# First MLP of an attention and two-MLP kernel: its first products split into 64-row pairs, in two phases with the transposes of an older tile between them

## The reference

```python
# attention: 4 x 8 heads, 576 positions, 64 wide; a score below (max - tau) is dropped
scores = scale * q @ k.T
attn = softmax(where(scores >= max - tau, scores, -1e9))
x = (attn @ v) as 2304 x 512
# first MLP
h = x @ w_in                            # 2304 x 1024
sm = exp(h - max(h)) / (sum + 1e-9)
solu = h * sm
ln = (solu - mean) / sqrt(var + 1e-6) * g_ln
y = ln @ w_out                          # 2304 x 512
# second MLP
h = y @ w_in2                           # 2304 x 2048
out = (max(h, 0) + log1p(exp(-abs(h)))) @ w_out2
```

## Time and profile before

| | |
|---|---|
| Median of 3 runs | 888.11 us (887.92 to 888.94) |
| The profiled execution, its own time | 887.9 us |
| Its span in the trace | 886.2 us |
| Granted TensorE clock, mean over the span | 0.998 |
| Busy: PE, PEld | 861.7 us (97%), 716.5 us (81%) |
| Busy: DVE, ACT, POOL | 638.6 us (72%), 567.1 us (64%), 324.3 us (37%) |
| Products h_ps of line 1040 | 432, in three groups of 144 |
| Transposes of line 1188 | 288 |
| The part with tiles 2 to 17 and their y_ps | about 275.7 to 463.0 us of the span |

### The profile page before, as it was taken

One profiled execution on the slowest core, in us unless ns is written; L12 is line 12 of the kernel. 1 busy time (PEld: TensorE's weight loads), 2 busy tenths in 40 slices (PEclk: granted clock), 3 DMA queues, 4 the chain that ended last, 5 costly groups with the idle time before them and its releaser, 6 DMA issues.

```text
span 886.2 us, 16881 instructions
## 1 busy us (share of the span) xinstructions
PE 861.7 (97%) x6248; PEld 716.5 (81%) x6248; DVE 638.6 (72%) x1286; ACT 567.1 (64%) x1040; POOL 324.3 (37%) x425
## 2 busy tenths in 40 slices
PE   6899999999999999999999999999999999999998
PEld 4566666666667889898899999999999999999996
DVE  6899999999955633615447578867858858868865
ACT  3787988787876533424356566666666667667664
POOL 3554677555544601102021232333332232233232
PEclk9999999999999999999999999999999999999999
DMA  6713423343001100000021500000100000000000
GB/s 167 205 47 81 110 55 75 88 108 108 18 1 37 37 1 1 2 1 1 1 84 49 178 1 1 37 0 1 37 1 1 37 1 1 36 0 0 36 0 36
DMA packets 30394, 37.16 MB, mean 42 GB/s; under 512 B 4720, under 2 KB 18544, under 8 KB 30320
## 3 DMA queue, kind: packets, MB, share of 16 engines
q1 hardware_dynamic: 29920, 35.90, 14.7%
q10 hardware_dynamic: 400, 0.30, 0.1%
HBM read 31.46 MB, written 4.72 MB: 41 GB/s over the span
## 4 chain that ended last, share of the span: by engine, by line
PE 55%; issue 25%; POOL 9%; DVE 9%; ACT 0%; DMA 0%; ACTq 0%; POOLq 0%; DVEq 0%
PE h_ps L1040 12%; PE y_ps L1176 11%; POOL w_lo L527 9%; PE m_ps L1152 8%; PE f_ps L1241 7%; DVE ntop L837 7%; PE s_ps L1072 7%; PE o_ps L1112 5%; PE t_ps L1088 2%; PE lt_ps L1188 1%; PE s_ps L1067 1%; DVE kept L853 1%; DVE inv L869 0%; PE l_ps L1083 0%; DMA k_sb<-k_t 0%
## 5 line engine op out<-in xcount | busy, mean ns | idle before, releaser
L1152 PE MATMUL m_ps<-y_hi,w 128*128 128x384 f32 x768 | 211.8, 337 | 0.0
L527 POOL TENSOR_TENSOR w_lo<-w_rest,w_hi 128x512 fp32r<-128x512 f32 x84 | 110.3, 1313 | 253.5 <-ACT w_hi L700 253.4
L1152 PEld LDWEIGHTS m_ps<-y_hi,w 128*128 128x128 f32 x768 | 140.3, 188 | 3.9
L580 ACT ACTIVATE expd<-s_ps,ntop 128x576 f32<-128x576 f32 x144 | 106.2, 741 | 51.6 <-DVE ntop L837 51.6
L1152 PE MATMUL m_ps<-y_lo,w 128*128 128x384 f32 x384 | 129.0, 336 | 0.0
L700 ACT CAST w_hi<-w_rest 128x512 fp32r<-128x512 f32 x84 | 52.2, 622 | 109.1 <-PE f_ps L1241 105.7
L465 POOL TENSOR_SCALAR kept<-kept,inv 128x576 f32<-128x576 f32 x144 | 105.8, 750 | 38.8 <-DVE inv L869 38.7
L837 DVE TENSOR_REDUCE ntop<-s_ps 128x1 f32<-128x576 f32 x144 | 107.4, 757 | 14.3 <-PE s_ps L1072 8.3
L1241 PE MATMUL f_ps<-w_hi,g_hi 128*128 128x512 f32 x288 | 113.4, 394 | 0.7 <-POOL w_lo L527 0.7
L966 DVE SCALAR_TENSOR_TENSOR g<-u,z 128x384 f32<-128x384 f32 x96 | 53.2, 554 | 84.1 <-ACT u L716 84.1
L1241 PE MATMUL f_ps<-w_hi,g_lo 128*128 128x512 f32 x288 | 113.8, 395 | 0.0
(11 more groups left out here) (89 smaller groups left out, 1650.5 us busy)
## 6 DMA issues: line engine op xcount, KB each, us to landing
q_sb<-q_t SPq DMA_DIRECT2D x28, 288.0 KB, 5.2
v_sb<-v_main SPq DMA_DIRECT2D x16, 256.0 KB, 3.2
stage<-w_in SPq DMA_DIRECT2D x16, 256.0 KB, 2.7
out<-o_sb SPq DMA_DIRECT2D x5, 768.0 KB, 3.6
w_rest<-w_out SPq DMA_DIRECT2D x7, 512.0 KB, 5.4
k_sb<-k_t SPq DMA_DIRECT2D x21, 144.0 KB, 4.6
stage<-w_in SPq DMA_DIRECT2D x4, 512.0 KB, 8.1
stage<-w_out SPq DMA_DIRECT2D x4, 512.0 KB, 6.3
```

Source lines behind the costliest of these rows:

```text
L527: nc.gpsimd.tensor_tensor(w4[1][n % 2], w4_rows(n % F2, 1)[:, 0, :], f32(w4[0][n % 2]), ALU.subtract).then_inc(w4lo_made, 1)
L580: nc.scalar.activation(expd[:, tile % 2, :].rearrange("p (a b) -> p a b", a=2), s_ps[tile % 2][:, :, 0:HALF], ACT.Exp, bias=ntop[:, tile % ...
L1152: last = nc.tensor.matmul(m_ps[n % 4][:, 0:GC], w[n % F2][:, k, :], y[odd][:, k, :], start=(k == 0 and m == 0), stop=(k == C - 1 and m == 2))
```

## The change

`mlp1` on PE no longer calls `hidden` for tiles 2 to 17, but a new function `hidden_half` twice: phase 0 before the transposes of tile-2, and phase 1 behind them. Each product of 128 rows becomes two of 64 rows, `q` = 0 and 1, on the two halves of the array. In phase 0 the lower half of the rows makes the first 512 columns and the upper half the last 512; in phase 1 it is the other way round, and is added to the same banks. A phase has 24 products of 64 rows, a tile 48 instead of 24 of 128 rows. h_made is raised by the last of phase 1. A new semaphore h_half is raised by the last product of phase 0 and waited for ahead of phase 1. The waits for x_lo and solu stay ahead of phase 0, the waits of the transposes stay ahead of them, and so stand between the phases now. `project` stands behind phase 1. Nothing changes on the other engines.

```diff
+        h_half = sem("h_half")
...
+            def hidden_half(tile, slot, phase):
+
+                if phase == 1:
+                    pe.wait_ge(h_half, tile - 1)
+                for k in range(C):
+                    for n, (x, w) in enumerate(((x_hi, w1[0]), (x_hi, w1[1]), (x_lo, w1[0]))):
+                        for q in range(2):
+                            side = slice((q ^ phase) * BANK, (q ^ phase) * BANK + BANK)
+                            last = nc.tensor.matmul(h_ps[slot][:, side], x[halves[q], slot, k, :], w[halves[q], k, side],
+                                                    start=(phase == 0 and k == 0 and n == 0),
+                                                    stop=(phase == 1 and k == C - 1 and n == 2))
+                last.then_inc((h_half, h_made)[phase], 1)
+
...
             def mlp1(i, n):
                 tile = 6 * i + n
-                if within(tile, MT) and not (isinstance(i, int) and i == 0 and n < 2):
+                new = within(tile, MT) and not (isinstance(i, int) and i == 0 and n < 2)
+                if new:
 
                     pe.wait_ge(xlo_made, tile + 1)
                     wait(pe, solu_made, tile - 1)
-                    hidden(tile, n % 2)
+                    hidden_half(tile, n % 2, 0)
...
                     transpose_row(tile, n % 2)
+                if new:
+                    hidden_half(tile + 2, n % 2, 1)
                 if (n - 5) % GROUP == 0:
```

## The result

The changed kernel takes 939.27 us (median of 4 runs, 938.57 to 940.79), the kernel before took 888.01 beside it: a ratio of 1.0586, 95% interval 1.0565 to 1.0607. The forecast was 934.3 with a range of 917 to 947, and a chance of 0.96 that the kernel gets slower. The profiled execution took 940.79 us, its span is 939.0 us.

What follows compares the result with a forecast made beforehand. In the first MLP the prediction took PE to bound the kernel, every PE wait counting in full. From 887.9 us, +33.2 for stops and y_ps tiles and +13.2 for the falling clock gave 934.3 us, range 917 to 947.

Steps and rivals of the forecast that it cites:

- The pairs at 0.233: First MLP on PE: a pair of 64-row products takes 0.233 us, bounds 0.213 to 0.467; a tile's products stay 5.60 us.
- 980: Rival, first MLP: the two products of a pair don't overlap, adding 59 us for 980 us; chance 0.05.
- 948: Rival, first MLP: next pair's weights wait for the running pair, 27 us on 921, giving 948 us; chance 0.03.
- The turns: Around the transposes: no turns left between 128-row and 64-row work, so a tile away from y_ps would take 6.15, not 6.44 us.
- The stop, which decided: PE waits about 3.1 us for ln_lo before the transposes in 11 tiles; 9.39 us per tile, 32.5 us in all.
- the wake-up on the semaphore: PE's restart after ln_lo ends, before the transposes: taken as 0.10 us, bounds 0 and 0.27.
- The tiles at y_ps: Tiles behind y_ps and tile 2: h 0.81 us later, 4.0 in all; y_ps sooner after the products, 3.3 less.
- The other waits at nothing: First MLP: waits for ln, h_half, x_lo and solu cost nothing; no DMA or other queue is moved.
- The sum up to here: Stops 32.5 plus later tiles 4.0 minus earlier y_ps 3.3: +33.2 us, 921.1 us before any clock cost.
- The clock, mis-sized: PE's clock falls to half after most of 11 stops, 1.2 us each, bounds 0 and 1.7: +13.2 us.
- the rival of a half clock through whole tiles: Half clock lasts through the 11 stopping tiles, 2.9 us each, 32 on top of 921: 953 us; chance 0.05.
- the rival "not slower": ln_lo is free before VectorE turns to the next tile, so PE isn't stopped and only turns count: 885.4 us; chance 0.03.

Runs made afterwards that it cites:

- with the clock held: Changed kernel plus 11 unused pairs of 64-row products into idle y_ps banks after phase 0 in the 11 stopping tiles; 921.27 us, 1.0372 of before.
- order alone: Changed kernel's two phases around the transposes, but with the 128-row products of before, one half of the columns per phase; 941.13 us, 1.0599 of before.
- pairs alone: Changed kernel's 64-row pairs, but with both phases before the transposes; 890.13 us, 1.0025 of before.
- with ln_lo in time: Changed kernel, PE untouched; ScalarE and VectorE make ln_hi and ln_lo for the tile one before, except behind y_ps; 885.38 us, 0.9972 of before.
- the kernel with ln_lo first: Changed kernel, PE untouched; ln_hi and ln_lo of the tile two before made ahead of x_hi and the maximum; 889.45 us, 1.0028 of before.

## Why the prediction held, and where its numbers were off

1. **The pairs at 0.233.** Measured 0.233 in the changed kernel, both starts together. The 64 x 288 scores of the earlier trace rows stood in for a product that the trace didn't have, and they proved less than the working says: 0.24 for a pair is also what two products of 288 columns at 2.4 GHz would take one after the other, and no row shows what one half takes alone. The value was right; it is the 0.233 for 512 columns, above the 0.213 of one half alone and far from 0.467, that shows the overlap. Both rivals on it (980, 948) fall.
2. **The turns.** 6.15 expected for a tile without them, 6.14 measured once nothing else was in the way.
3. **The stop, which decided.** Expected about 3.1 us in 11 tiles, measured 2.97 to 3.07 in 11 tiles. The step between two h was forecast at 9.39 and is 9.35 with the clock held; the wake-up on the semaphore takes 0.05 (ln_lo ends at 345.98, the transposes start at 346.03), not the 0.10 that I took.
4. and 5. **The tiles at y_ps.** The maximum of the tile behind y_ps was to come 0.81 - 0.65 = 0.16 later than the 23.10 of before; with the clock held it comes after 23.24.
6. **The other waits at nothing.** Right: the wait of lt_ps for ln_lo is the only new one of PE in the stage. The sum up to here was +33.2, the run with the clock held has +32.9 in the stage and takes 921.3 against the 921.1 of the working.
7. **The clock, mis-sized.** Forecast 1.2 a stop, 13.2 in all; measured 18.9 in all, 1.7 a stop. It fell in all 11. Two things make the difference. First, the slow stretch falls almost wholly on work that the kernel waits for: in nine of the eleven it begins within 0.8 us of the stop's end (346.02 against 346.03 in the tile shown), in the others 1.0 before and 1.5 behind it. Nine stretches of 3.4 us cost 1.3 to 1.55 us each against the same tiles with the clock held, 13.5 together; I had let part of each fall on P0, where it costs nothing. Second, in two of the eleven it lasted 6.8 us: those tiles took 11.94 and 12.12 us in place of 10.6 to 11.0, 2.6 and 2.8 more than with the clock held, 5.3 together. The upper bound of the working, 3.4 / 2 = 1.7, holds for the short stretches only; the long ones cost what the rival of a half clock through whole tiles put at 2.9, which I had given a chance of 0.05 for all tiles and none for some. The 1.31 us of the earlier trace rows was the price of one product group in such a stretch, not of a whole one.

The remaining 1.1 us of the profiled execution is attention's, with the longer early fall of the clock, which I had not put in. The mechanism was forecast in all its steps; 934.3, the clock's 5.7 more, 0.3 less in the other terms and these 1.1 make the 940.8 of the profiled execution, and the median is 1.5 below that.

The failed rivals are told apart by one experiment each: order alone costs all of it (941.1), pairs alone next to nothing (890.1), the clock is 18.9 us of it (921.3), and the rival "not slower" named the right mechanism, since with ln_lo in time the kernel takes 885.38, and that rival had been put at 885.4 (that the two agree so closely is luck, as attention alone varies by a microsecond). It was wrong only in that the change as made doesn't touch VectorE's order.

## What to carry to other kernels

When work is put between two halves of a step, look at the waits in front of that work, not at its length: they had a whole step to be met in, and now have half of one, and the engine that meets them may itself be waiting for the other half. A reordering on one engine wants the same reordering on those that feed it; here the same PE order is 51 us slower or 2.5 us faster than before, by where two instructions stand on ScalarE and VectorE. Judge such a move over a whole period and not by one tile: a maximum nearly 2 us late was made good by the next. A stop of a few microseconds that recurs on TensorE should be priced with the fall of the clock that follows it, in full.

## What the runs showed of the hardware

- Two fp32r products of 64 rows and 512 columns, on the two halves of the array, take the 0.233 us of one of 128 rows. Their weights load under the running pair: those of the pair of 342.42 from 342.18, when the pair before had just started. A turn from 128-row to 64-row work and back costs about 0.3 us around the transposes (6.44 against 6.14 for a tile).
- Eleven idles of 3.0 us each dropped the granted clock to 0.5 in 11 of 11 cases (and again in 11 of 11 with 128-row products), eleven of 1.8 to 1.9 us in 8 of 11, eleven of 1.1 to 1.2 us in none, nor did the two of 1.4 us in the kernel with ln_lo first. I had not expected that the same idle of 1.8 us goes either way in one run, nor that two of the falls (three with 128-row products) would last 6.8 instead of 3.4 us.
- The early fall in attention differs between executions of the same code: none, 3.4, 6.8 or 10.2 us in the ten profiled ones, with the maximum of tile 1 at 274.4, 275.8 to 276.0, 276.9 and 276.7 to 277.0 us. Single whole runs can't show a microsecond; the stage can.
- Filling an idle with products that nobody reads made the kernel 18 us faster (939.27 to 921.27).
- A second phase that a semaphore holds until the last product of the first is finished starts 0.46 instead of 0.23 us behind that product's start, if nothing stands between them. Whether the sums would come out right without the semaphore was not tried.
